# Attention and mixer on one core: channel weights and x loaded in portions, x's tail turned over 128 partitions, and another order of work at the handover

## The reference

```python
q_rot, k_rot = rotate(q), rotate(k)
scores = scale * q_rot @ k_rot.T
attn = exp(scores - max) / (sum + 1e-09)
attn_out = attn @ v                        # (4, 8, 576, 64)
x = attn_out.transpose(0, 2, 1, 3).reshape(4, 576, 512)
h = relu(x.T @ w_tok1) @ w_tok2
u = x + h.T
out = u + relu(u @ w_ch1) @ w_ch2
```

## Time and profile before

| what | value |
|---|---|
| median of three runs | 685.3 us (683.94 to 687.86) |
| profiled execution: time | 682.41 us |
| profiled execution: span from first to last instruction | 680.6 us |
| mean granted clock of TensorE | 0.995 |
| TensorE busy | 645.8 us, 95% |
| VectorE, ScalarE, GpSimd busy | 465.6, 410.1, 251.3 us |

### The profile page before, as it was taken

How to read it: one execution, slowest core, us unless ns; L and a number is a source line. 1 busy time by engine, 2 the same in 40 slices (tenths; PEclk the granted TensorE clock), 3 DMA queues, 4 the chain that set the end, 5 groups by cost and what they waited for, 6 DMA issues and landing times.

```text
span 680.6 us, 13572 instructions
## 1 busy us (share of the span) xinstructions
PE 645.8 (95%) x4848; PEld 625.1 (92%) x4848; DVE 465.6 (68%) x823; ACT 410.1 (60%) x916; POOL 251.3 (37%) x250
## 2 busy tenths in 40 slices
PE   1799999999997999998999999999999999999996
PEld 1689999999897999997999999999989999999996
DVE  5799999999896999976375872128830367512484
ACT  3488888888886899985273653226532245422453
POOL 1998888888785888460900000000000000000000
PEclk9999999999998999999999999999999999999999
DMA  8566656658678664406000031000210002100001
GB/s 227 140 159 153 154 151 156 155 151 205 166 243 202 155 156 119 118 19 204 18 1 1 1 102 47 1 1 1 78 69 0 0 0 77 70 1 1 1 1 70
DMA packets 60121, 60.88 MB, mean 89 GB/s; under 512 B 18848, under 2 KB 45088, under 8 KB 60064
## 3 DMA queue, kind: packets, MB, share of 16 engines
q1 hardware_dynamic: 60064, 60.12, 32.8%
HBM read 28.64 MB, written 9.44 MB: 56 GB/s over the span
## 4 chain that ended last, share of the span: by engine, by line
PE 88%; SPq 3%; DVE 3%; ACT 2%; DMA 2%; issue 1%; POOL 0%; ACTq 0%; POOLq 0%; DVEq 0%
PE slot L535 11%; PE rest L568 10%; PE rest L545 8%; PE slot L1106 7%; PE slot L1104 7%; PE slot L1105 7%; PE rest L1106 7%; PE rest L1104 7%; PE rest L1105 7%; PE rest L579 3%; PE rest L510 2%; PE slot L1137 2%; PE rest L1137 2%; PE rest L555 2%; DMA q_cross<-t_hi_q 2%; PE rest L218 1%
## 5 line engine op out<-in xcount | busy, mean ns | idle before, releaser
L1337 DVE TENSOR_TENSOR pieces<-h,pieces 128x288 fp32r<-128x288 f32 x168 | 75.0, 453 | 88.6 <-ACT pieces L1257 88.3
L849 DVE TENSOR_REDUCE neg_max<-slot 128x1 f32<-128x576 f32 x144 | 107.9, 750 | 12.7 <-PE slot L535 7.9
L1257 ACT ACTIVATE pieces<-h 128x288 fp32r<-128x288 f32 x168 | 74.5, 444 | 46.5 <-PE rest L1106 23.3
L857 DVE TENSOR_TENSOR pt_lo<-rest,pt_hi 128x512 fp32r<-128x512 f32 x144 | 95.9, 676 | 2.3 <-ACT pt_hi L743 1.6
L743 ACT ACTIVATE pt_hi<-rest 128x512 fp32r<-128x512 f32 x144 | 83.9, 595 | 11.3 <-PE rest L545 10.8
L568 PE MATMUL rest<-pt_hi,v 128*128 128x256 f32 (+1 forms) x320 | 89.5, 303 | 0.0
L535 PE MATMUL slot<-key,q_hi 128*128 128x288 f32 x256 | 65.6, 338 | 15.5 <-DMA q_cross<-t_hi_q 11.7
L568 PE MATMUL rest<-pt_lo,v 128*128 128x256 f32 (+1 forms) x256 | 69.9, 295 | 0.0
L736 ACT ACTIVATE prob_a<-slot,neg_max 128x576 f32<-128x576 f32 x80 | 59.3, 742 | 16.3 <-DVE neg_max L849 16.1
L568 PEld LDWEIGHTS rest<-pt_hi,v 128*128 128x128 f32 x320 | 60.4, 189 | 0.0
L1350 DVE TENSOR_TENSOR h<-h 128x288 f32<-128x288 f32 x96 | 41.6, 451 | 24.8 <-ACT h L1239 24.4
(11 more groups left out here) (180 smaller groups left out, 1858.7 us busy)
## 6 DMA issues: line engine op xcount, KB each, us to landing
key<-t_hi_k SPq DMA_DIRECT2D x32, 144.0 KB, 2.3
key<-t_lo_k SPq DMA_DIRECT2D x32, 144.0 KB, 2.5
raw_qk<-in_k_dram SPq DMA_DIRECT2D x16, 256.0 KB, 2.9
raw_qk<-in_q_dram SPq DMA_DIRECT2D x16, 256.0 KB, 2.7
q_hi<-t_hi_q SPq DMA_DIRECT2D x32, 128.0 KB, 2.4
q_cross<-t_lo_q SPq DMA_DIRECT2D x32, 128.0 KB, 2.4
q_cross<-t_hi_q SPq DMA_DIRECT2D x32, 128.0 KB, 2.4
raw_v<-in_v_dram SPq DMA_DIRECT2D x16, 256.0 KB, 2.8
```

The costliest lines, as they stand in the source:

```text
L849: dve.tensor_reduce(neg_max[p % 2][:, i:i + 1], slot[g % 2][:, :, 0:HALF], AX.XY, ALU.max, negate=True).then_inc(maxed, 1)
L857: dve.tensor_tensor(pt_lo[:, :, cols], rest[:, bank, :].rearrange("p (j n) -> p j n", j=G), f32(pt_hi[:, 0:G, cols]), ALU.subtract).then_i ...
L1257: act.activation(pieces[:, ring(m), 0, :], source[WEIGHTS[n]][:, ft, :], ACT.Copy).then_inc(piece_hi, 1)
L1337: dve.tensor_tensor(pieces[:, ring(m), 1, :], source[WEIGHTS[n]][:, ft, :], f32(pieces[:, ring(m), 0, :]), ALU.subtract).then_inc(piece_lo, 1)
```

## The change

- `ChannelWeights.load` sends for half of a quarter (384 KB). The eight pieces are issued one each at the end of pairs 2 to 9.
- The x of batch 0 is sent for in three portions, at the end of pairs 10, 11 and 12: groups 0 and 1, groups 2 and 3, both tails.
- ScalarE makes the hidden values' high part of batch 0 (`first_token_hi`) inside the attention's program, behind the weights' seventh piece and ahead of the last copy of B's output; it waits for a new semaphore, `sums_ready`, that the last token product raises.
- `Q` becomes (1, 0, 2, 3): the second unit of u takes slot 0, the third slot 2, the fourth slot 3.
- VectorE makes the weights' last low part behind the low part of the second unit of u.
- The tail of x is turned as a tile of 128 partitions with 128 columns, instead of 64 and 64. The columns added hold the tail a second time and are not read.

```diff
@@ ChannelWeights
-    def load(self, sp, w_ch1, c):
-        sp.dma_start(self.arrived[:, c, :], w_ch1[c * P:(c + 1) * P, :]).then_inc(self.loaded, 16)
+    def load(self, sp, w_ch1, c, half):
+        cols = slice(half * CH // 2, (half + 1) * CH // 2)
+        sp.dma_start(self.arrived[:, c, cols], w_ch1[c * P:(c + 1) * P, cols]).then_inc(self.loaded, 16)
...
@@ attention, sync: loop over p
-            if p == N - 8:
-
-                sp.wait_ge(x_stored, STORED * (p - 2))
-                sp.wait_ge(w_lo_done, len(chunks))
-                token.load_x(sp, 0)
-            if p == N - 6:
-                for c in range(CT):
-                    w1.load(sp, w_ch1, c)
             store(p - 2)
...
             assemble_q(1, p + 1)
+            if 2 <= p < 2 + 2 * CT:
+                w1.load(sp, w_ch1, (p - 2) // 2, p % 2)
+            if p == 10:
+
+                sp.wait_ge(x_stored, STORED * HP)
+                sp.wait_ge(w_lo_done, len(chunks))
+                token.load_x(sp, 0, range(0, 2), ())
+            if p == 11:
+                token.load_x(sp, 0, range(2, HP), ())
+            if p == 12:
+                token.load_x(sp, 0, ())
@@ attention, tensor
-        token.products(pe, 0, 4, first)
+        token.products(pe, 0, 4, first).then_inc(token.sums_ready, 1)
@@ attention, scalar
         w1.split_hi(act, 3, 0)
+        act.wait_ge(token.sums_ready, 1)
+        h1_of_batch_0(act)
         copy_o(p - 1, "B1")
         w1.split_hi(act, 3, 1)
@@ attention, last_sums
-        w1.split_lo(dve, 3)
@@ mixer
-    Q = (1, 2, 3, 0)
+    Q = (1, 0, 2, 3)
@@ mixer, u_unit
-                if c < 3:
+                if Q[c] > 0:
                     first.slot_left(pe, Q[c])
...
-                n, rows_ = (P, P) if t < G else (TAIL, TAIL)
                 f, at = (0, t * P) if t < 2 else (1, (t - 2) * P)
-                pe.matmul(s[:, f, at:at + n], xn[0:n, t, cols], ident[0:n, 0:n], start=(t in (0, 2)), stop=False,
+                pe.matmul(s[:, f, at:at + P], xn[:, t, cols], ident[:], start=(t in (0, 2)), stop=False,
                           is_transpose=True, skip_group_check=True)
@@ mixer, scalar
-        token_hi(slot[0])
@@ mixer, vector
                 u_lo(b, c)
+                if begins and c == 1:
+                    w1.split_lo(dve, 3)
```

More of the change, by code:

```diff
@@ L127, in _ @@
                 def _(act):
-                    first.scalar(act)
+                    first.scalar(act, then.first_token_hi)
                     then.scalar(act)
@@ L137 @@
 Attention = namedtuple("Attention", "sync gpsimd tensor scalar vector last_o last_sums last_store buffers_left values_left slot_left")
-Mixer = namedtuple("Mixer", "sync gpsimd tensor scalar vector")
+Mixer = namedtuple("Mixer", "sync gpsimd tensor scalar vector first_token_hi")
 class ChannelWeights:
@@ L147, in __init__ @@
                                                    for n in ("loaded", "hi_done", "lo_done"))
-    def load(self, sp, w_ch1, c):
-        sp.dma_start(self.arrived[:, c, :], w_ch1[c * P:(c + 1) * P, :]).then_inc(self.loaded, 16)
+    def load(self, sp, w_ch1, c, half):
+        cols = slice(half * CH // 2, (half + 1) * CH // 2)
+        sp.dma_start(self.arrived[:, c, cols], w_ch1[c * P:(c + 1) * P, cols]).then_inc(self.loaded, 16)
     def split_hi(self, act, c, half):
         if c == 0 and half == 0:
-            act.wait_ge(self.loaded, 16 * CT)
+            act.wait_ge(self.loaded, 2 * 16 * CT)
         cols = slice(half * CH // 2, (half + 1) * CH // 2)
@@ L181, in __init__, with load_x @@
         self.x_hi_done, self.x_lo_done = sem("x_hi_done"), sem("x_lo_done")
-        self.x_used = sem("x_used")
-    def load_x(self, sp, b):
+        self.x_used, self.sums_ready = sem("x_used"), sem("sums_ready")
+    def load_x(self, sp, b, groups=range(HP), tails=(0, TAIL)):
         x = self.x_scratch.rearrange("(b g) s c -> b g s c", g=HP)[b]
-        for g in range(HP):
+        for g in groups:
             sp.dma_start(self.xn[:, 0:G, g * P:(g + 1) * P],
                          x[g][0:MAIN, :].rearrange("(p t) c -> p t c", t=G)).then_inc(self.x_in, 16)
-        for r in (0, TAIL):
+        for r in tails:
             sp.dma_start(self.xn[r:r + TAIL, G, :].rearrange("p (g c) -> p g c", g=HP),
@@ L716, in slot_left, with scalar @@
             pe.wait_ge(o_summed["B"], N)
-    def scalar(act):
+    def scalar(act, h1_of_batch_0):
         def t_part_hi(n, p, bank):
@@ L1217, in ready, with token_hi @@
         eng.wait_ge(unit_ready, b * UNITS + k)
+    def token_hi(act, s):
+        for a in range(TT):
+            act.activation(h1[0][:, a, :], s[:, a, :], ACT.Relu).then_inc(h1_hi_done, 1)
     def scalar(act):
-        def token_hi(s):
-            for a in range(TT):
-                act.activation(h1[0][:, a, :], s[:, a, :], ACT.Relu).then_inc(h1_hi_done, 1)
         def u_hi(b, c):
@@ L1303, in body @@
                 ready(act, b, CT + HIDDEN + 2)
-                token_hi(slot[TOK])
+                token_hi(act, slot[TOK])
             copy_rows(b, 1, last)
@@ L1468, in vector @@
         body(B - 1, last=True)
-    return Mixer(sync=sync, gpsimd=gpsimd, tensor=tensor, scalar=scalar, vector=vector)
+    return Mixer(sync=sync, gpsimd=gpsimd, tensor=tensor, scalar=scalar, vector=vector, first_token_hi=lambda act: token_hi(act, slot[0]))
 _INS = ['q', 'k', 'v', 'moe_w_tok1', 'moe_w_tok2', 'moe_w_ch1', 'moe_w_ch2']
```

## The result

The changed kernel takes 668.5 us (median of six runs, 667.3 to 669.4), against 685.5 us of the kernel before measured as often; the ratio is 0.9748, with a 95% interval from 0.9729 to 0.9767. The profiled execution of after has a time of 669.35 us and a span of 667.6 us, against 682.41 and 680.6: there the difference is only 13.1 us. So most of what was missed is a distance between single executions and medians, and the experiments look for its cause.

The account below looks back on a forecast made before the run. TensorE, holding 88% of the chain of waits, was taken as the bound. Loads 6.6, handover 4.0 and tails in batches 1 to 3 3.2 sum to 13.8 us: 685.3 - 13.8 = 671.5 us, range 669 to 676.5.

Parts of the forecast that it names:

- the two waits in the loop: Attention loop: TensorE stands 1.09 us before the score at 175.24 and 3.52 us before the one at 213.62.
- the two at the handover: Start of the mixer: TensorE waits 1.78 us for the token layer's low part, then 1.10 us for head A's sum.
- rival of the forecast: Five: wide tail gains nothing 10%, small DMAs delay 10%, handover gives first wait only 9%, long pairs' other cause 3%, slower 3%.
- Weights and x: Attention loop: loads sent in small portions cost 0 and remove the 5.23 and 1.36 us of two long pairs.
- Tails: Mixer, turning of x: a 128-partition tail gains 0.27 us a unit, 3.2 us in batches 1 to 3, 0.8 in batch 0.
- Handover: From attention to mixer, batch 0: first hidden unit starts at 327.2 instead of 331.17, 4.0 us with its tails.
- the last step of the sum: Whole kernel: the median stays 2.9 us above the profiled execution, so 685.3 - 13.8 = 671.5 us.
- The two long pairs: Attention loop: pairs of 18.65 and 22.52 us against an undisturbed 17.29, 6.59 us together, caused by the moved loads.
- bound for the x block: Attention loop: one x portion costs between 0 and 0.5 us, a third of the block's 1.36; taken as 0.
- the wait of 3.52 us: Attention loop, before the score at 213.62: matmul pairs behind it take 0.85 instead of 0.53 us; that pair loses 5.23 us.
- the 1.78 us one: Handover, after turning x at 317.18: TensorE waits for the hidden values' low part; products start 1.85 us earlier.
- The moved low part of the weights: Mixer, behind the second u unit: 1.76 us of VectorE, hidden by the fourth unit's 2.2 us; cost 0, bound 1.8.

## Why the prediction was right and wrong

**Right.** *What bounds it and where the gaps are:* the two waits in the loop and the two at the handover went, and no rival of the forecast appeared at its price. *Weights and x:* 6.6 us forecast, 6.9 as the sum of two kernels and 7.2 together; the pieces cost 0, with a wide margin. *Tails:* 4.0 us forecast with those of batch 0, 3.9 measured, 0.46 us as taken. *Handover:* the steps came out as worked out. ScalarE's activations began at 309.24, that is 0.73 us ahead of TensorE's turning of x (0.68 forecast), the products followed 0.63 us after it began (0.7 forecast), the second unit 3.42 us (3.5), the hidden unit 9.84 us (10.0). The sum of parts against the profiled execution was 13.8; the traces of before and after differ by 13.0 in their spans.

**Wrong: the last step of the sum.** It read: the median is 2.9 us above the profiled execution, "I leave this distance as it is". That treated the distance as a constant that both kernels have. It belongs in part to the very stalls that the change takes out, and so two terms of the sum were too small: by the runs the handover without the tails gives 4.6 us for 3.2, the loads 6.9 to 7.2 for 6.6, though neither difference alone is beyond its interval. Of the 3.3 us missed (17.1 - 13.8):
- The two long pairs are 6.6, 8.3, 7.3 and 6.9 us over in four profiles of the kernel before, 7.3 on average. The first of the four had the lowest, though with the handover alone changed it was 5.0, and over all seven profiles with both blocks in their old places the average is 6.9. So 0.3 to 0.7 us were missed. The forecast had a bound for the x block and none for the burst from above; it took one execution's price as the price. The burst's wait hardly varies (3.24 to 3.88 us in eight profiles); the one pair of 23.81 us has twice the time at the lower clock.
- The clock behind the handover's wait costs 1.4 us where it falls, in 4 of 6 profiles, 0.9 us on average if those six profiles are typical. The forecast looked for the clock's level behind the wait of 3.52 us and priced it. For the 1.78 us one, behind which the first trace has full speed, it did not ask whether this was always so.
- 0.9 us is chance in the first samples: 1.3 us from that of before (685.5 against the 684.2 of 71 runs), less 0.4 us the other way from that of after (668.5 against 668.1 of 11).
- These make 2.1 to 2.5 us. What is left, 0.8 to 1.2 us, no run here separates; it is inside the intervals of the experiments.

The profile of the changed kernel made the distance between the two gains (17.1 and 13.1 us) larger, since it errs the other way: its 669.35 us is the longest of its eleven runs, with about 1.0 us of waits at 480 to 482 us that the next profile does not have. With 16.1 us by all runs, the forecast was 2.3 us short and the range a little too high at its low end: its lower bound had 1.5 us for the runs' spread, and it should have had the spread on top of the costs of stalls that can be larger than once seen.

**A cover that was nearly lost.** The moved low part of the weights was put at 1.76 us, and at no cost even if the third low part of u slipped by all of it. VectorE's and GpSimd's timelines in the changed kernel, and GpSimd's in the kernel before:

```profile
317.21 3.42 DVE L164 TENSOR_TENSOR w_ch_lo<-w_ch_whole,w_ch_hi 128x1536 fp32r<-128x1536 f32 x1
320.56 1.54 DVE L1326 TENSOR_TENSOR ut_lo<-rest,ut_hi 128x256 fp32r<-128x256 f32 x4
315.52 8.49 POOL L1094 TENSOR_TENSOR w_ch_S_whole<-w_ch_A_whole 128x1536 f32<-128x1536 f32 x2
...
326.05 6.97 POOL L1089 TENSOR_TENSOR w_ch_S_whole<-w_ch_A_whole 128x1536 f32<-128x1536 f32 x2
```

It takes 3.42 us where GpSimd's sums of the second weights run beside it, and two of those take 8.49 us instead of 6.97 (3.32 and 8.49 us in the next profile). The third low part ends at about 321.3, and TensorE begins the step that needs it at 321.42; its second product follows after 0.24 us instead of the usual 0.13. So it costs about 0.1 us (0.05 in the next profile), and the cover is used up. That the step was of no cost was nearly right, the 1.76 us was not. The Trainium skill, "GPSIMD Engine Reference", Specifications, says that GpSimd shares its SBUF interfaces with VectorE and contends with VectorE instructions that have two inputs in SBUF, the memory that also holds the weights. This one has two, and the trace agrees; the low part of the second unit, with one input in the accumulator memory, took its usual 0.82 us at 316.47 beside the same sums.

**Open.** Why the clock falls behind the same 1.8 us wait in some executions and not in others, and whether the burst has a part in it: 4 of 6 profiles against 0 of 4 is a pattern, not a proof, and the clocks of the single runs do not bear it out as a rule.

## What to carry to other kernels

Where a change removes a stall, the distance between the profiled execution and the median is not a constant: look at two or three executions, and let the upper bound of a stall be its longest one. A block of loads on a queue that also feeds the bounding engine should go where that queue has its longest time to the next thing needed. Here 1.5 MB in two DMAs were free at the end of a pair, and 1.25 MB in six DMAs, which hold SP for 3.9 us, cost up to 1.9 us ahead of the store; the runs do not tell the place from the number of DMAs. 3.1 MB in one go cost about 5 us at either place. A transpose of a tile with half the partitions can cost more than that of a whole one.

## What the runs showed of the hardware

A 64-partition transpose between full ones costs 0.26 to 0.27 us more than a full one, though it has half the columns, and its weight load begins 0.17 us late; one of the form 128*64 costs no more than a full one. A wait of TensorE of 1.77 us can be followed by 3.4 us of lower clock, at a price of 1.4 us, and the same wait in the same place may not be. So can one of 3.24 to 3.88 us, as in eight of eight profiles, while behind one of 2.94 us the clock stayed at its full level. VectorE's subtraction of 128x1536 took 1.76 us alone and 3.42 us beside GpSimd's sum of two SBUF tiles.
